# Token tiles for the channel stage turned by VectorE 32x32 blocks instead of TensorE transposes, with a new order at the stage's entry

## The chip, the core and the metric

One core of a Trainium2 chip. Time is device microseconds of the core, the median of three runs. The profile is of one execution, and its span runs from the first to the last instruction.

## What is computed

Windowed attention over 2 batches, 8 heads, 768 tokens, head size 64; then a gated unit (`w_in` 512x1024, a 768x768 product over tokens, `w_out` 512x512); then a low-rank token mix and a channel network (512 to 2048 to 512) with a residual:

```python
attn = softmax(scale * q @ k.T + bias, kept in the window) @ v     # -> x: 2 x 768 x 512
h = relu(x @ w_in); u, v = h[..., :512], h[..., 512:]
x2 = (u * (w_spatial @ layer_norm(v) + b_spatial)) @ w_out
u = x2 + (x2.T @ U @ V).T                                          # low rank, 32
out = u + relu(u @ w_ch1) @ w_ch2
```

All in float32. The kernel splits each operand of a large product in a high and a low part (`hi`, `lo`, type fp32r) and adds three products: hi by hi, lo by hi, hi by lo.

## The kernel before

Tokens lie in 12 tiles of 128 (6 of each batch), 512 columns each, in the SBUF tensor `tokens`. The engines run programs of their own, in an order written out by hand, and meet by semaphores. `wait(e, name, n)` adds a credit that the waiting side's buffers give.

Attention and the gated unit of batch 0 come first (`window`), then the in-products and layer norm of batch 1, then `finish`, which begins with `products(1)`: for each of its six tiles t TensorE runs `mix_tokens` (18 matmuls), six transposes of the next row of `w_spatial`, `low_rank(t-2)`, `project(t-1)` (12 matmuls), and the four transposes of the gated tile (`gate_transpose`, L1266). VectorE in the same period does `gate` (L957), two `wsp_lo`, `x2_lo(t-1)`, `gT_lo`; ScalarE the copies with the high parts. The gate of tile t must be done before `gate_transpose(t)`; `gT_lo(t)` before `project(t)`, one period later; `x2_lo(t)` before `low_rank(t)`, two periods later.

The channel stage works on groups of TB = 4 tiles, so there are NB = 3 groups. Each group needs its four tiles turned (`uT`, columns on partitions), split in `uT_hi` and `uT_lo`. Then it goes in NF = 16 steps: `hidden(n)` makes 128 of the 2048 hidden columns (12 matmuls of 512), ScalarE and VectorE split the result in `hT_hi` (L719) and `hT_lo` (L1094), and `down(n)` adds it into four y banks (12 matmuls). TensorE runs `hidden(n+1)` ahead of `down(n)`, and there are two buffers of h. After a group's last step VectorE adds y and tokens into `ys` (`y_out`, L1099), and SyncE stores it.

Before the change the tiles are turned in `u_transpose` (L1414): four TensorE transposes of a tile into one of two PSUM banks (2 and 3), then `uT_hi` on ScalarE (L712) and `uT_lo` on VectorE (L1089), both from PSUM. The first group's are set between the last products of batch 1: tiles 0 and 1 after `gate_transpose(5)`, tiles 2 and 3 after `project(5)`, and `hidden(0)` waits for all four. The second group's are set between `down(14)` and `down(15)`, the third's one group later. The third transpose of a group waits until the first bank has been split by both engines. The tokens of batch 1 are complete only after `add_low_rank(1, t)` (L983), which runs in the first steps of the first group, from `expand` (L1291).

Meanwhile GpSimd splits the channel weights (`split_chunk`, L402: a cast L408 and a subtraction L410 of 128x1024 for each chunk): eight chunks from 235 us on, the other eight after the last `gate`.

All of TensorE's products are at L1156, all its transposes at L1148, the two low-rank products at L1287, the expansion at L1297.

## Time and profile before

| | us |
|---|---|
| median of 3 runs | 570.76 |
| the three runs | 568.64, 570.76, 573.37 |
| the profiled execution | 568.82 |
| its span | 566.9 |
| TensorE busy in it | 532.1 (94%) |
| VectorE busy in it | 233.3 (41%) |
| ScalarE busy in it | 172.4 (30%) |
| GpSimd busy in it | 111.7 (20%) |

The granted TensorE clock is at full speed (2.4 GHz) in every one of the page's 40 slices. The channel stage runs from about 292 us to the end. A matmul of 128x512 shows about 390 ns in the trace, but back to back one starts every 0.227 us: matmuls are pipelined, so the starts tell the pace and the busy time does not. The same holds of VectorE on a smaller scale: a group of two rows can be shorter than twice the mean.

### The profile page before, as it was taken

To read this page: it belongs to the slowest core of one execution; us is meant where nothing else is said; L and a number is where in the kernel's file an instruction comes from. 1 tells how busy PE (TensorE), PEld (TensorE's weight loads), DVE (VectorE), ACT (ScalarE), POOL (GpSimd) and SP (SyncE) were. 2 spreads that over 40 slices of the span, in tenths; PEclk is the share of its full clock that TensorE was granted. 3 is DMA by queue.
4 is the path that set the end of the run, shared out by engine and by line. 5 is a ranking of instruction groups with operands and counts; after the bars stand their busy time and mean duration, and the time that the engine had idled before them with its cause. 6 is when DMAs were issued, how large, how long until landed. Compare 5 with 4: busy or idle time off the path is not lost.

```text
span 566.9 us, 7455 instructions
## 1 busy us (share of the span) xinstructions
PE 532.1 (94%) x2724; PEld 415.3 (73%) x2724; DVE 233.3 (41%) x656; ACT 172.4 (30%) x426; POOL 111.7 (20%) x134
## 2 busy tenths in 40 slices
PE   1789999889999999999979999999999999999996
PEld 0356666567777788778868888878888887888885
DVE  5668888867775436533343110123010114110112
ACT  2655665655555432223141011121011012011110
POOL 3786000000000001599299200000000000000000
PEclk9999999999999999999999999999999999999999
DMA  8995443545623000055133000001000002000002
GB/s 168 221 223 129 99 101 102 120 96 129 127 77 90 29 29 0 6 179 182 43 111 112 1 0 1 0 1 74 1 0 1 0 1 75 1 0 1 0 1 79
DMA packets 43977, 37.02 MB, mean 65 GB/s; under 512 B 25600, under 2 KB 37888, under 8 KB 43936
## 3 DMA queue, kind: packets, MB, share of 16 engines
q1 hardware_dynamic: 37920, 20.13, 16.3%
q0 software_dynamic: 3216, 11.63, 6.8%
q10 hardware_dynamic: 2800, 4.72, 2.9%
q8 instruction: 24, 0.39, 0.3%
q14 instruction: 17, 0.14, 0.1%
HBM read 33.33 MB, written 3.15 MB: 64 GB/s over the span
## 4 chain that ended last, share of the span: by engine, by line
PE 84%; DVE 5%; SPq 4%; issue 3%; DMA 2%; ACT 1%; POOL 0%; DVEq 0%; ACTq 0%; POOLq 0%
PE ps L1156 68%; PE ps L1148 6%; PE ps L1171 4%; PE ps L1196 4%; SPq L337 2%; DMA qk_even<-in_k 1%; PE ps L1287 1%; DMA wsp<-in_moe_w_spatial 1%; SPq L371 1%; DVE pr L869 1%; SPq L373 1%; DVE sc L853 1%; DVE gv_lo L937 1%; DVE q_turned L805 1%; POOL small L447 0%
## 5 line engine op out<-in xcount | busy, mean ns | idle before, releaser
L1096 DVE SCALAR_TENSOR_TENSOR hT_lo<-ps,hT_hi 128x512 fp32r<-128x512 f32 x48 | 33.2, 692 | 211.6 <-ACT hT_hi L722 211.6
L722 ACT ACTIVATE hT_hi<-ps 128x512 fp32r<-128x512 f32 x48 | 28.7, 598 | 224.9 <-PE ps L1156 224.9
L549 ACT ACTIVATE pr<-sc,small 128x256 f32<-128x256 f32 (+1 forms) x96 | 46.2, 482 | 52.9 <-DVE small L853 52.4
L1171 PE MATMUL ps<-k_turned,q_turned 64*128 64x256 f32 (+1 forms) x192 | 36.4, 460 | 16.4 <-DVE k_turned L805 10.0
L853 DVE CUSTOM_DVE_ANT_0 sc<-ps,bias 128x256 f32<-128x256 f32 (+1 forms) x96 | 34.9, 399 | 20.9 <-PE ps L1171 17.8
L1156 PE MATMUL ps<-win_hi,xT_hi 128*128 128x512 f32 x96 | 40.2, 419 | 0.0
L1156 PE MATMUL ps<-uT_hi,w1a_hi 128*128 128x512 f32 x96 | 37.5, 390 | 2.3 <-issue 2.3
L1156 PE MATMUL ps<-win_hi,xT_lo 128*128 128x512 f32 x96 | 37.7, 393 | 0.0
L1156 PE MATMUL ps<-w2b_hi,hT_hi 128*128 128x512 f32 x96 | 37.6, 392 | 0.0
L1156 PE MATMUL ps<-win_lo,xT_hi 128*128 128x512 f32 x96 | 37.5, 391 | 0.0
L1156 PE MATMUL ps<-w2b_hi,hT_lo 128*128 128x512 f32 x96 | 37.4, 390 | 0.0
L1156 PE MATMUL ps<-w2b_lo,hT_hi 128*128 128x512 f32 x96 | 37.4, 390 | 0.0
L1156 PE MATMUL ps<-uT_lo,w1a_hi 128*128 128x512 f32 x96 | 37.4, 390 | 0.0
L1156 PE MATMUL ps<-uT_hi,w1a_lo 128*128 128x512 f32 x96 | 37.4, 390 | 0.0
L1156 PE MATMUL ps<-w2a_lo,hT_hi 128*128 128x512 f32 x96 | 37.4, 390 | 0.0
L1156 PE MATMUL ps<-uT_hi,w1b_hi 128*128 128x512 f32 x96 | 37.4, 390 | 0.0
L1156 PE MATMUL ps<-uT_lo,w1b_hi 128*128 128x512 f32 x96 | 37.4, 390 | 0.0
L1156 PE MATMUL ps<-w2a_hi,hT_lo 128*128 128x512 f32 x96 | 37.4, 389 | 0.0
L1156 PE MATMUL ps<-uT_hi,w1b_lo 128*128 128x512 f32 x96 | 37.4, 389 | 0.0
L1156 PE MATMUL ps<-w2a_hi,hT_hi 128*128 128x512 f32 x96 | 37.4, 389 | 0.0
L1171 PEld LDWEIGHTS ps<-k_turned,q_turned 64*128 64x128 f32 x192 | 16.6, 211 | 26.0 <-DVE k_turned L805 10.0
L1148 PE MATMUL ps<-ident,pr 128*128 128x128 f32 x176 | 31.3, 301 | 3.8 <-issue 2.5
(144 smaller groups left out, 1052.8 us busy)
## 6 DMA issues: line engine op xcount, KB each, us to landing
w_raw<-in_moe_w_ch POOLq DMA_DIRECT2D x16, 512.0 KB, 4.1
wsp<-in_moe_w_spatial ACTq DMA_DIRECT2D x12, 384.0 KB, 3.3
vn<-in_v SPq DMA_DIRECT2D x12, 256.0 KB, 3.8
out<-ys SPq DMA_DIRECT2D x12, 256.0 KB, 2.3
qk_late<-in_q SPq DMA_DIRECT2D x24, 112.0 KB, 3.6
qk_late<-in_k SPq DMA_DIRECT2D x24, 112.0 KB, 3.8
vp<-in_v SPq DMA_DIRECT2D x10, 224.0 KB, 4.6
w_raw<-in_moe_w_in POOLq DMA_DIRECT2D x4, 512.0 KB, 7.5
```

What stands on the lines that cost most here:

```text
L337: e.dma_start(qk_in(tile)[rows, a, :, :, :].rearrange("p a n d -> p a (n d)"), src[head, tile // NT, tile % NT, :, :, x * TURN:(x + SPAN) ...
L371: sp.dma_start(vp[0:P - G, buf, :, :], v_d[b, i - 1, G:P, :, :]).then_inc(s[f"v_loaded{buf}"], 16)
L373: sp.dma_start(vp[P - G:P, buf, :, :], v_d[b, 0, 0:G, :, :]).then_inc(s[f"v_loaded{buf}"], 16)
L549: act.activation(pr[:, k % 3, e, 0:w], sc[:, k % 2, e, 0:w], ACT.Exp, bias=nmax[:, k % 2, e:e + 1], scale=-1.0, accum_out=sums[:, k % 3, e ...
L722: act.activation(hT[0][:, n % 2, :], h1_ps(n), ACT.Relu).then_inc(s["hT_hi"], 1)
L805: ins = dve.transpose(out.rearrange("p a (r c) -> p a c r", c=TURNS), qk_in(tile)[:, a, :, 0:SPAN:2, :])
L853: dve.tensor_tensor_reduce(out=sc[:, k % 2, e, 0:w], in0=scores_ps(e)[:, 0:w], in1=bias[:, 2 * p + e, WINDOW - w:WINDOW], scale=-SCALE, sc ...
L1096: dve.scalar_tensor_tensor(hT[1][:, n % 2, :], h1_ps(n), 0.0, hT[0][:, n % 2, :], ALU.max, ALU.subtract).then_inc(s["hT_lo"], 1)
L1148: return pe.transpose(dst, src, ident[:, :])
L1156: ins = pe.matmul(o, lhsT[a], r[c], start=first_of_bank and (a, c) == (0, 0), stop=last and (a, c) == (1, 0))
L1171: pe.matmul(scores_ps(e)[:, 0:w], q_turned[rows, tile % 2, p, :], keys[:, window_at(i):window_at(i) + w]).then_inc(s["scores"], 1)
L1196: ins = pe.matmul(x_ps(tile)[e * D:(e + 1) * D, p * P:(p + 1) * P], v[:, buf, 2 * p + e, :], probs[:, e, x * P:(x + 1) * P], start=x == 0, ...
```

## The change

The 48 TensorE transposes of `tokens` and the function `u_transpose` are gone. In their place VectorE runs `turn_tokens(n, x)`: for one block of 32 token partitions (x) it makes four block transposes, each from 32 partitions and 4 x 32 columns into another block of 32 partitions, so that four calls, 16 instructions, turn a tile of 128x512 wholly, from SBUF to SBUF. The turned float32 tile lies in `turned(n)`: for the first group in the place of `uT_lo`, for the other two in `ys[j]`. `uT_hi` and `uT_lo` now read it there instead of in PSUM.

When: the first group's four tiles in `products(1)`, periods t = 0 to 3, half of a tile ahead of `x2_lo(t-1)` and half behind `gT_lo(t)`; the second and third group's during the steps f = 5 to 12 of the group before, two calls (8 instructions) behind each `hT_lo`. ScalarE's `uT_hi` of the first group goes into periods 1 to 4, VectorE's `uT_lo` behind `gT_lo` of periods 2 to 5.

The order of TensorE at the entry becomes `low_rank(4)`, `hidden(0)`, `project(5)`, `hidden(1)`, `low_rank(5)`, `down(0)`, then the usual steps; the first `down` waits with its fourth column block for `mix_lo`, whose bank it takes over (y_ps 3 is now bank 1). `expand` and `add_low_rank` of batch 1 come one step later. `y_out` also waits for `uT_lo` of the next group, since both use `ys`; a turn of the third group waits for the store of the first group's output from the same buffer.

```diff
--- before.py
+++ after.py
...
+FIRST_TURN = 5
...
         uT = hi_lo("uT", [P, CM, TB * P])
+        uT_end = place[0]
+        place[0] = uT_at + CM * TB * P * 4
+        uT_first = sb("uT_first", [P, CM, TB * P])
+        assert place[0] == uT_end
...
-        def uT_ps(j):
-            return ps[:, 2 + j % 2, :]
+        def turned(n):
+
+            j = n % TB
+            return ys[j][:, :].rearrange("p (c n) -> p c n", c=CM) if n >= TB else uT_first[:, :, j * P:(j + 1) * P]
...
         def y_ps(j):
-            return ps[:, (0, 1, 5, 6)[j], :]
+            return ps[:, (0, 5, 6, 1)[j], :]
...
+            def uT_hi(tb, j):
+                if j == 0:
+                    wait(act, "h1_ps", tb * NF)
+                act.wait_ge(s["u_turned"], tb * TB + j + 1)
+                act.activation(uT[0][:, :, j * P:(j + 1) * P], turned(tb * TB + j), ACT.Copy).then_inc(s["uT_hi"], 1)
...
                     gT_hi(b, t)
+                    if b and 0 < t <= TB:
+                        uT_hi(0, t - 1)
...
-            def uT_hi(tb, j):
-                if j == 0:
-                    wait(act, "h1_ps", tb * NF)
-                wait(act, "u_transposed", tb * TB + j + 1)
-                act.activation(uT[0][:, :, j * P:(j + 1) * P], uT_ps(j).rearrange("p (c n) -> p c n", c=CM),
-                               ACT.Copy).then_inc(s["uT_hi"], 1)
...
             def finish():
                 products(1)
-                for j in range(2):
-                    uT_hi(0, j)
+                hT_hi(0)
                 x2_hi(1, NT - 1, True)
-                for j in range(2, TB):
-                    uT_hi(0, j)
-                hT_hi(0)
+                hT_hi(1)
                 mix_hi(1, True)
-                for n in range(1, NB * NF):
+                for n in range(2, NB * NF):
                     hT_hi(n)
...
+            def turn_tokens(n, x):
+
+                tb, j = n // TB, n % TB
+                wait(dve, "u_ready", n + 1)
+                if tb > 1:
+                    dve.wait_ge(s[f"stored{j}"], 16 * (tb - 1))
+                rows = tokens[x * TURN:(x + 1) * TURN, n, :].rearrange("p (c y r) -> p c y r", y=TURNS, r=TURN)
+                for y in range(TURNS):
+                    ins = dve.transpose(turned(n)[y * TURN:(y + 1) * TURN, :, x * TURN:(x + 1) * TURN], rows[:, :, y, :])
+                if x == TURNS - 1:
+                    ins.then_inc(s["u_turned"], 1)
+
+            def uT_lo(tb, j):
+                n = tb * TB + j
+                dve.wait_ge(s["uT_hi"], n + 1)
+                dve.tensor_tensor(uT[1][:, :, j * P:(j + 1) * P], turned(n), uT[0][:, :, j * P:(j + 1) * P],
+                                  ALU.subtract).then_inc(s["uT_lo"], 1)
+
             def products(b):
                 for t in range(NT):
                     gate(b, t, True)
                     for h in range(2):
                         if t + 1 < NT:
                             wsp_lo(b, t + 1, h, True)
+                    for x in range(2):
+                        if b and t < TB:
+                            turn_tokens(t, x)
                     if t:
                         x2_lo(b, t - 1, True)
                     gT_lo(b, t)
+                    for x in range(2, TURNS):
+                        if b and t < TB:
+                            turn_tokens(t, x)
+                    if b and t >= 2:
+                        uT_lo(0, t - 2)
...
-            def uT_lo(tb, j):
-                dve.wait_ge(s["uT_hi"], tb * TB + j + 1)
-                dve.tensor_tensor(uT[1][:, :, j * P:(j + 1) * P], uT_ps(j).rearrange("p (c n) -> p c n", c=CM),
-                                  uT[0][:, :, j * P:(j + 1) * P], ALU.subtract).then_inc(s["uT_lo"], 1)
...
                 if m >= TB:
                     dve.wait_ge(s[f"stored{j}"], 16 * (m // TB))
+                if m + TB < B * NT:
+                    dve.wait_ge(s["uT_lo"], m + TB + 1)
                 dve.tensor_tensor(ys[j][:, :], y_ps(j), tokens[:, m, :], ALU.add).then_inc(s["y_ready"], 1)
 
             def finish():
                 products(1)
-                for j in range(2):
-                    uT_lo(0, j)
+                hT_lo(0)
                 x2_lo(1, NT - 1, True)
-                for j in range(2, TB):
-                    uT_lo(0, j)
-                hT_lo(0)
                 mix_lo(1, True)
                 for n in range(1, NB * NF):
                     hT_lo(n)
-                    if n <= NT // 2:
-                        add_low_rank(1, 2 * n - 2)
-                        add_low_rank(1, 2 * n - 1)
-                    tb = (n + 1) // NF
-                    if n % NF == NF - 1:
+                    if 2 <= n <= NT // 2 + 1:
+                        add_low_rank(1, 2 * n - 4)
+                        add_low_rank(1, 2 * n - 3)
+                    tb, f = n // NF + 1, n % NF
+                    if tb < NB and FIRST_TURN <= f < FIRST_TURN + 2 * TB:
+                        for x in range(2):
+                            g = 2 * (f - FIRST_TURN) + x
+                            turn_tokens(tb * TB + g // TURNS, g % TURNS)
+                    if f == NF - 1:
...
                     if f == 0 and tb:
                         wait(pe, "y_ready", (tb - 1) * TB + j + 1)
+                    if n == 0 and j == TB - 1:
+                        wait(pe, "mix_split", B)
...
-            def u_transpose(tb, j):
-                n = tb * TB + j
-                wait(pe, "u_ready", n + 1)
-                wait(pe, "uT_lo", n - 1)
-                for c in range(CM):
-                    ins = transpose(uT_ps(j)[:, c * P:(c + 1) * P], tokens[:, n, c * P:(c + 1) * P])
-                ins.then_inc(s["u_transposed"], 1)
-
             def finish():
                 wait(pe, "u_ready", NT)
                 products(1)
                 wait(pe, "wspT_lo", 2 * B * NT)
-                for j in range(2):
-                    u_transpose(0, j)
                 low_rank(1, NT - 2, True)
+                hidden(0)
                 project(1, NT - 1, True)
-                for j in range(2, TB):
-                    u_transpose(0, j)
-                wait(pe, "gate", B * NT)
-                hidden(0)
+                hidden(1)
                 low_rank(1, NT - 1, True)
-                for n in range(NB * NF):
-                    tb = (n + 1) // NF
+                down(0)
+                for n in range(1, NB * NF):
                     if n + 1 < NB * NF:
                         if n % NF == NF - 1:
-                            for j in range(TB):
-                                u_transpose(tb, j)
                             down(n)
                             hidden(n + 1)
                             continue
                         hidden(n + 1)
-                    if n < NT // 2:
-                        expand(1, 2 * n)
-                        expand(1, 2 * n + 1)
+                    if n <= NT // 2:
+                        expand(1, 2 * n - 2)
+                        expand(1, 2 * n - 1)
                     down(n)
```

## Rows read from the trace of the kernel before

**Rows 1.** The page: busy time by engine, and the chain's shares of the span.

```profile
PE 532.1 (94%) x2724; PEld 415.3 (73%) x2724; DVE 233.3 (41%) x656; ACT 172.4 (30%) x426; POOL 111.7 (20%) x134
...
PE 84%; DVE 5%; SPq 4%; issue 3%; DMA 2%; ACT 1%; POOL 0%; DVEq 0%; ACTq 0%; POOLq 0%
```

**Rows 2.** Chain of waits at the second and third group: start us, us, what.

```profile
378.52 0.45 PE ps L1148 x4
...
381.74 87.11 PE ps L1156 x384
468.85 0.45 PE ps L1148 x4
...
472.35 89.81 PE ps L1156 x396
```

**Rows 3.** Chain of waits at the entry to the channel stage, same columns.

```profile
285.33 0.73 PE ps L1287 x2
...
289.83 2.27 issue
292.10 3.00 PE ps L1156 x12
295.10 0.45 PE ps L1287 x2
...
298.73 5.44 PE ps L1156 x24
```

**Rows 4.** Timeline of VectorE, 43 to 46 us: start us, us, engine, line, operation.

```profile
43.87 1.11 DVE L805 STREAM_TRANSPOSE q_turned<-qk_odd 128x512 f32<-128x512 f32 x1
44.82 1.10 DVE L805 STREAM_TRANSPOSE k_turned<-qk_odd 128x512 f32<-128x512 f32 x1
```

**Rows 5.** Groups of VectorE by form: xcount, busy us, mean ns, idle before.

```profile
L933 DVE TENSOR_SCALAR small<-small 128x1 f32<-128x1 f32 x12 | 1.8, 154 | 0.4
L937 DVE TENSOR_TENSOR gv_lo<-vnf,gv_hi 128x512 fp32r<-128x512 f32 x12 | 9.6, 800 | 1.7 <-ACT gv_hi L601 1.7
L980 DVE TENSOR_TENSOR mix<-ps,mix 32x512 fp32r<-32x512 f32 x2 | 1.4, 684 | 0.8 <-ACT mix L629 0.7
```

**Rows 6.** Timeline of VectorE, 237 to 286 us: the product stage of batch 1.

```profile
237.35 2.08 DVE L937 TENSOR_TENSOR gv_lo<-vnf,gv_hi 128x512 fp32r<-128x512 f32 x1 [0.70 <-ACT gv_hi L601]
...
246.46 0.75 DVE L964 SCALAR_TENSOR_TENSOR gated<-ps,small,gu 128x512 f32<-128x512 f32 x1 [3.13 <-PE ps L1156]
...
255.06 0.75 DVE L964 SCALAR_TENSOR_TENSOR gated<-ps,small,gu 128x512 f32<-128x512 f32 x1 [2.16 <-PE ps L1156]
255.91 1.02 DVE L956 TENSOR_TENSOR wspT_lo<-ps,wspT_hi 128x384 fp32r<-128x384 f32 x2
260.02 0.69 DVE L974 TENSOR_TENSOR x_lo<-ps,x_hi 128x512 fp32r<-128x512 f32 x1 [3.09 <-ACT x_hi L625]
...
285.19 0.68 DVE L969 TENSOR_TENSOR gT_lo<-ps,gT_hi 128x512 fp32r<-128x512 f32 x1
```

**Rows 7.** Timeline of GpSimd in the same stretch, same columns.

```profile
236.45 2.43 POOL L410 TENSOR_TENSOR w1a_lo<-w_raw,w1a_hi 128x1024 fp32r<-128x1024 f32 x1
...
266.81 1.05 POOL L408 CAST w2a_hi<-w_raw 128x1024 fp32r<-128x1024 f32 x1
267.94 2.40 POOL L410 TENSOR_TENSOR w2a_lo<-w_raw,w2a_hi 128x1024 fp32r<-128x1024 f32 x1
...
285.48 1.05 POOL L408 CAST w1b_hi<-w_raw 128x1024 fp32r<-128x1024 f32 x1
```

**Rows 8.** Chain of waits, 255 to 264 us: one tile of the product stage.

```profile
255.02 0.66 PE ps L1148 x6
...
256.14 2.73 PE ps L1156 x12
...
263.43 0.66 PE ps L1148 x6
```

**Rows 9.** Timeline of VectorE in the channel stage, 376 to 378 us.

```profile
376.46 0.69 DVE L1096 SCALAR_TENSOR_TENSOR hT_lo<-ps,hT_hi 128x512 fp32r<-128x512 f32 x1 [4.75 <-ACT hT_hi L722]
```

More of the change, by code:

```diff
@@ L63 @@
               pT_ready=2, av=1, xT_hi=1, xT_lo=2, d_xT_lo=3, v_relu=2, u_relu=2, wsp_transposed=1, wspT_lo=2, gate=2,
-              gT_lo=1, x2_split=2, low_rank=2, mix_split=1, h_ps=1, u_ready=2, u_transposed=1, uT_lo=2, h1_ps=1,
+              gT_lo=1, x2_split=2, low_rank=2, mix_split=1, h_ps=1, u_ready=2, h1_ps=1,
               hT_lo=2, h2=2, y_ready=4, d_bias=0)
@@ L201, in program @@
         place[0] = turned_at
+        uT_at = place[0]
         uT = hi_lo("uT", [P, CM, TB * P])
+        uT_end = place[0]
+        place[0] = uT_at + CM * TB * P * 4
+        uT_first = sb("uT_first", [P, CM, TB * P])
+        assert place[0] == uT_end
         hT = hi_lo("hT", [P, 2, TB * P])
@@ L292, in program @@
             x2_sum x2_hi x2_split low_rank mix_hi mix_split h_ps u_ready
-            u_transposed uT_hi uT_lo h1_ps hT_hi hT_lo h2 y_done y_ready""".split()}
+            u_turned uT_hi uT_lo h1_ps hT_hi hT_lo h2 y_done y_ready""".split()}
         def wait(e, name, n):
@@ L749, in _ @@
             give(dve, "qk_turned", "bias_ready", "biased", "normal", "xT_lo", "d_xT_lo", "wspT_lo", "gate", "gT_lo",
-                 "x2_split", "mix_split", "u_ready", "uT_lo", "hT_lo", "y_ready")
+                 "x2_split", "mix_split", "u_ready", "hT_lo", "y_ready")
             steps = [0]
@@ L1141, in _ @@
             give(pe, "low_rank", "scores", "probsT", "av", "wsp_transposed", "h_ps",
-                 "u_transposed", "h1_ps", "h2")
+                 "h1_ps", "h2")
             pe.wait_ge(s["dense_ready"], 1)
```

## The prediction

> **What bounds the kernel now.** I read the busy times of the page first, then the chain of waits over the second half of the span, then the timeline of each engine at the three places where tiles are turned. The busy times show TensorE at 532 of 567 us, VectorE at 233, and the chain lies on TensorE for 84% of the span [rows 1]. So an edit is worth what it takes off TensorE's own line or out of its idle time, and VectorE's added work costs nothing as long as it stays in VectorE's gaps. In the channel stage the chain is nothing but matmuls one behind another for 87 us between groups [rows 2]; it is broken only where tiles are turned. Those three places are the whole possible gain.
>
> **What is removed at the second and third group.** The chain leaves the matmuls at 378.52 and is back on them at 381.74, 3.22 us; at the next group 468.85 to 472.35, 3.50 us [rows 2]. Both stretches are the 16 transposes and a wait for the first PSUM bank to be split. After the change TensorE goes from `down(14)` to `down(15)` to `hidden(16)` with nothing between, if `uT` is ready. Is it? After `hidden(15)` the h split ends with `hT_lo` at 376.46 + 0.69 = 377.15 [rows 9]. Four `uT_lo` behind it, at 0.68 each and each fed by a ScalarE copy that is no slower, end by about 380; `hidden(16)` would start 12 matmuls (2.73, as in a `project` [rows 8]) behind 378.52, at 381.25. A margin of 1.2 us, so I take the whole 3.22 + 3.50 = 6.7 us as saved. The `y_out` that follow are needed only two products later.
>
> The turning itself puts 8 block transposes behind each `hT_lo` in steps 5 to 12. A step is 24 matmuls, 5.44 us [rows 3]; `hT_lo` takes 0.69 of it. The cover holds up to a price of (5.44 - 0.69) / 8 = 0.59 us for each block transpose; above it `hT_lo` falls back from step to step and `down` waits.
>
> **What one block transpose costs.** The trace has none of 32 partitions by 128 columns. The nearest are those of 128x512: 1.11 us long, and the next starts 0.95 behind [rows 4]. Fewer partitions give no rebate: a subtraction on 32 partitions took 0.684, as much as on 128 [rows 5, 6]. By columns: the lower bound is a quarter of the start distance, 0.24 us. If an instruction of one column takes 0.154 [rows 5] and the rest of 1.11 goes by columns, the length is 0.154 + 0.24 = 0.39. As a top I take 0.44, that length and a hand-over of 0.05 between two. The choice between 0.24 and 0.39 is whether the next one overlaps the tail of the one before. The transposes of the trace that overlap write the same partitions; the new ones change their output block with each instruction. I take 0.39.
>
> The Trainium skill, VectorE: DVE Perf Modes, section "Two Vector instructions with no wait between them", says that an instruction whose output starts in another group of 32 partitions than the one before begins only when all earlier ones have finished. No row of before shows such a pair; by that rule the overlap is gone in all 192 instructions, and the price is at or above the full length. The same page's section "The three transpose paths" gives 311 ns for 128 columns of 16-bit data and advises TensorE for a full 128x128 transpose; by its figure the entry below would come out as in the cheap case, about -9 in all.
>
> **The entry, without VectorE's load.** In before the chain ends `down(0)` 2.72 into the piece that starts at 298.73, at 301.45, of which 0.45 are two expansions that now come later: 301.0 [rows 3]. After: `low_rank(4)` still waits for `x2_lo(4)` until 285.33, now idle, and ends at 285.8. `hidden(0)` waits for `uT_lo(3)`, which stands behind `gT_lo(5)` (to 285.87 [rows 6]). That subtraction now has two SBUF inputs, and here is a cost that it did not have from PSUM: `gv_lo` of the same shape, started during a GpSimd subtraction, took 2.08, where the other eleven have a mean of (9.6 - 2.08) / 11 = 0.68 [rows 5], and ended 0.55 behind that instruction's end [rows 6, 7]. GpSimd's cast runs from 285.48 to 286.53 [rows 7], so `uT_lo(3)` ends at 287.1. Then `hidden(0)` 2.75, `project(5)` 2.73, `hidden(1)` 2.73, `low_rank(5)` 0.47, `down(0)` 2.72: 298.5. `mix_lo` is done by about 297.3 and its user is the last quarter of `down(0)`, at 297.8. Saving 2.5 us. Of the old waits, 2.27 us ahead of 292.10 and a short one ahead of 285.33, the latter stays and grows by the eight transposes that filled its front, and 1.3 us are left ahead of `hidden(0)`.
>
> **VectorE's load in `products(1)`.** A period is 8.41 us (255.02 to 263.43 [rows 8]). VectorE's work in it is `gate` 0.75, `wsp_lo` 1.02, `x2_lo` 0.69, `gT_lo` 0.68, and from the third period on `uT_lo` 0.68: 3.8 us. Added in periods 0 to 3: 16 block transposes, 3.8 us at 0.24, 6.2 at 0.39, 7.0 at 0.44. So up to 0.28 the period holds them (3.8 + 4.5 = 8.3); at 0.39 it is overfull by 1.6 in a period with `uT_lo`. What comes late is the next `gate`, queued behind the turns, and TensorE waits for it at `gate_transpose`, 0.66 + 0.45 + 2.73 = 3.84 behind the end of `mix_tokens` [rows 3, 8], less 0.75 for the gate: 3.1 us of slack. Step by step at 0.39 (one half turn 3.1 us):
> - t=1: gate at 249.1 instead of 246.46, done 249.9, TensorE needs it at 250.4. `wsp_lo` to 250.8, half turn, `x2_lo` to 254.5, `gT_lo` to 255.1, half turn.
> - t=2: gate at 258.2 instead of 255.06, done 258.9: TensorE loses up to 0.3. Then half turn, `x2_lo` to 263.6, `gT_lo` to 264.2, half turn to 267.3, and `uT_lo(0)` meets the cast of 266.81 to 267.86 [rows 7] and ends at 268.4.
> - t=3: gate 268.4 to 269.1: TensorE loses 1.7. The same again, without a GpSimd instruction in the way: `uT_lo(1)` to 278.0.
> - t=4: gate done 278.7: loses 1.2. No turns any more; by t=5 nothing waits.
>
> Sum of losses 3.2, and GpSimd's second half, started by the last gate, shifts along with it. The entry is then -2.5 + 3.2 = about +0.8 us (with rounding). Total: -6.7 + 0.8 = **-5.9 us**. Against the profiled span 566.9 that is 561.0; laid on the median of before, 570.76, it is 564.9. The profiled execution (568.82) lies 1.9 below that median, and I assume the same pace for after.
>
> Hidden and at no cost: ScalarE's `uT_hi` from SBUF (ScalarE is idle for 70% of the span [rows 1]), the waits of `y_out` for `uT_lo` (long done, same engine), those of the turns for the stores (three quarters of a group earlier), the swap of y banks.
>
> **The rivals.**
> - Cheap block transposes (price at most 0.36): losses in the products vanish or stay under 1 us; the entry gives -2.5 to -1.6 and the total is -9.3 to -8.4, so 561.5 to 562.4. For it: the start distance of rows 4. Against: outputs in other partitions each time.
> - Dear ones (0.41 to 0.48). The same walk at 0.44 loses 0.5, 1.4, 2.6 and 2.0 us, above all because `uT_lo(0)` now falls in the GpSimd subtraction of 267.94 to 270.34 [rows 7] and drags the gate behind it. Entry +4.0, total -2.7: 568.1. The skill's rule of the held instruction leads here if the hand-over is added to the length.
> - Slower than before: VectorE becomes the bound. From 0.50 the walk's loss (+7.3) eats the 6.7; from 0.59 the steps of the channel stage fall behind too. At 0.60 the entry loses some 13.7, total +7: 578. It needs a price above half of a four times longer one; little speaks for it.
> - The gain at the group boundaries doesn't come whole: `uT_lo` of the second group is later than `hidden(16)`, by more than the 1.2 us of margin, say because ScalarE's four copies come at 0.9 instead of 0.5 each. It would give back up to 2 us of each boundary: total -2, 568.9.
>
> **How the numbers follow.** Forecast case (price 0.37 to 0.40) 0.33, cheap 0.30, dear 0.27, boundaries late 0.05, slower 0.05. The three first are one mechanism at three prices, and the time forecast lies between them. A difference under 1%, 5.7 us, can't be told from no change here. Faster by over 1%: all of the cheap case and 0.25 of the forecast case, 0.55. Within 1%: the rest, 0.40. Slower 0.05. The range goes from the cheap case with 1 us for the spread of a median, 560.5, to the dear one with 2.7, 570.8.
>
> **What would show it.** Right: no transposes of `tokens` on TensorE, an unbroken chain of matmuls over both boundaries (each 3.2 to 3.5 shorter), block transposes starting 0.39 apart, the gates of t=3 and t=4 late by 1 to 2 us against TensorE, `hidden(0)` behind a `uT_lo` that ends after a GpSimd instruction. Wrong: block transposes under 0.3 or over 0.42 apart; `uT_lo` that is not held by GpSimd; a granted clock under full speed after one of the waits in the product stage, which before's gap of 2.27 us did not cause.

## The result and the profile after

| | before | after |
|---|---|---|
| median | 571.84 us (4 runs, 568.64 to 573.37) | 564.01 us (4 runs, 561.43 to 565.52) |
| span of the profiled execution | 566.9 | 559.6 |
| VectorE busy | 233.3 | 292.0 |
| TensorE busy | 532.1 | 525.5 |

The ratio is 0.9873 with a 95% interval of 0.9844 to 0.9902: 1.3% faster. The forecast was 564.9 us, a saving of 5.9; measured is a saving of 7.8 between these medians and of 7.3 between the two profiled spans.

The page of the kernel after, its parts 1 and 2 and one group of part 5 (busy us, mean ns of one | idle before):

```profile
PE 525.5 (94%) x2676; PEld 409.6 (73%) x2676; DVE 292.0 (52%) x848; ACT 172.2 (31%) x426; POOL 112.1 (20%) x134
...
PEclk9999999999999999999989999999999999999999
...
L1003 DVE STREAM_TRANSPOSE ys<-tokens 32x128 f32<-32x128 f32 x128 | 38.7, 302 | 1.8
```

VectorE has taken on 58.7 us of work, 192 block transposes at 0.302 us and little else, and the span fell all the same: the work went into its gaps. One digit of the clock is new, the 8 in the 21st slice, which is the entry to the channel stage. In [rows 1] the chain lay on TensorE for 84% of the span; now it is 80%, because it runs over VectorE in the products of batch 1. The chain of waits of after over 255 to 480 us (start us, us, what):

```profile
263.50 2.40 DVE uT_lo L1010
265.90 0.67 DVE gated L970
...
284.47 0.69 DVE x_lo L980
285.16 0.60 DVE gT_lo L975
285.76 1.21 DVE uT_lo L1010
...
287.01 10.09 PE ps L1185 x36
297.10 0.45 PE ps L1316 x2
297.55 5.44 PE ps L1185 x24
...
315.23 164.79 PE ps L1185 x727
```

Three things are to be read in it. The last row runs to the end of the window, at 480: where [rows 2] had 3.22 and 3.50 us of turning and waiting, matmuls now follow each other without a break. The first row is `uT_lo(0)`, which took 2.40 us instead of 0.68 and made a gate late. And `hidden(0)`, `project(5)` and `hidden(1)`, the 36 matmuls from 287.01, take 10.09 us where 36 at the usual distance of 0.227 take 8.2.

What TensorE waited for in after from 225 us on (us in total, times, longest):

```profile
PE ps L1316 <- DVE x_lo L980: 1.6, 1, 1.6
PE ps L1185 <- DVE gv_lo L943: 1.1, 1, 1.1
PE ps L1185 <- DVE uT_lo L1010: 1.0, 1, 1.0
PE ps L1177 <- DVE gated L970: 0.8, 2, 0.6
```

VectorE's timeline in the products of after, a few of its rows:

```profile
241.73 2.50 DVE L1003 STREAM_TRANSPOSE uT_first<-tokens 32x128 f32<-32x128 f32 x8
...
263.50 2.40 DVE L1010 TENSOR_TENSOR uT_lo<-uT_first,uT_hi 128x512 fp32r<-128x512 f32 x1
265.83 0.74 DVE L970 SCALAR_TENSOR_TENSOR gated<-ps,small,gu 128x512 f32<-128x512 f32 x1
...
285.68 1.28 DVE L1010 TENSOR_TENSOR uT_lo<-uT_first,uT_hi 128x512 fp32r<-128x512 f32 x1
```

and GpSimd's in the same stretch:

```profile
262.96 2.40 POOL L418 TENSOR_TENSOR w2a_lo<-w_raw,w2a_hi 128x1024 fp32r<-128x1024 f32 x1
...
285.35 1.05 POOL L416 CAST w1b_hi<-w_raw 128x1024 fp32r<-128x1024 f32 x1
```

Eight block transposes take 2.50 us: one is 0.302 long and they start 0.315 apart. Both slow `uT_lo` end 0.5 us behind the end of the GpSimd instruction (265.90 and 286.96 against 265.36 and 286.40), as `gv_lo` did before [rows 6, 7].

**Where the 7.3 us of the two spans lie.** In both kernels TensorE waits for `gv_lo` ahead of the last three matmuls of batch 1's first `mix_tokens`; the entry is counted from there, for all kernels below too, to the start of `down(0)`. Before took 239.49 to 298.73 [rows 3], less 0.45 for two expansions that come later now, so 58.8. After took 238.92 to 297.55, 58.6: the entry gained 0.2. From `down(0)` to the last matmul, with the two expansions counted alike, it gained 6.8, the 6.7 of the boundaries and 0.1; the end behind the last matmul took 0.25 longer. The other 0.6 us lie ahead of 239, where the two programs have the same work and single executions begin this stretch anywhere from 238.9 to 241.8. Part of that spread goes with the clock: the six of this document's fourteen profiles with a granted clock of 0.83 to 0.85 from 110 to 120 us begin it at 239.98 to 241.81, the other eight at 238.88 to 240.05.

Before's 58.8 holds a chance delay. This row of TensorE's timeline of before is a wait for a row of `w_spatial` to land:

```profile
246.84 0.88 PE L1148 MATMUL ps<-ident,wsp 128*128 128x128 f32 x6 [0.41 <-DMA wsp<-in_moe_w_spatial]
```

The other profiles of before (`before_b` and `before_c`, below) don't have it, nor has after; with the slower start behind it, it puts TensorE 0.65 us back by the next `project`. `before_c`, at full clock and without it, has an entry of 58.1. So the gain is the boundaries, and the entry is a wash: 0.2 us better than this execution, 0.5 worse than one without the late load. The questions for the chip were why, and whether it must be.

### The profile page after: what moved, and what is told of

Same layout as the page of the kernel before. It is cut to its first block, busy times and chain, and to the rows that moved or that the text cites. A ratio compares the mean times of both kernels' runs of the same rounds, so it can differ in the third digit from the quotient of the medians.

```text
span 559.6 us, 7557 instructions
## 1 busy us (share of the span) xinstructions
PE 525.5 (94%) x2676; PEld 409.6 (73%) x2676; DVE 292.0 (52%) x848; ACT 172.2 (31%) x426; POOL 112.1 (20%) x134
## 4 chain that ended last, share of the span: by engine, by line
PE 80%; DVE 9%; DMA 3%; POOL 3%; issue 3%; ACT 1%; SPq 0%; DVEq 0%; POOLq 0%; ACTq 0%
PE ps L1185 66%; PE ps L1177 5%; PE ps L1225 4%; PE ps L1200 4%; DMA w_raw<-in_moe_w_in 3%; DVE uT_first L1003 2%; POOL win_lo L433 2%; PE ps L1316 1%; DMA qk_even<-in_q 1%; POOL win_hi L431 1%; DVE pr L875 1%; DVE uT_lo L1010 1%; DVE wspT_lo L962 1%; DVE gv_lo L943 1%; DVE sc L859 1%
## 5 line engine op out<-in xcount | busy, mean ns | idle before, releaser
L1003 DVE STREAM_TRANSPOSE ys<-tokens 32x128 f32<-32x128 f32 x128 | 38.7, 302 | 1.8
```

The lines of the kernel that those rows point to most:

```text
L1003: ins = dve.transpose(turned(n)[y * TURN:(y + 1) * TURN, :, x * TURN:(x + 1) * TURN], rows[:, :, y, :])
```

## Experiments

The theories at this point. **Load:** VectorE's 64 block transposes in the products make gates late, by their price and by `uT_lo` meeting GpSimd. **Clock:** the two waits at the entry (1.6 and 1.0 us, with only the two matmuls of `low_rank(4)` between them) bring TensorE to its lower clock, and the next matmuls pay. The profile has a sign of it. TensorE's timeline of after behind the second wait:

```profile
288.58 0.63 PE L1185 MATMUL ps<-uT_lo,w1a_hi 128*128 128x512 f32 x1
289.01 0.63 PE L1185 MATMUL ps<-uT_hi,w1a_lo 128*128 128x512 f32 x1
289.43 0.63 PE L1185 MATMUL ps<-uT_hi,w1a_hi 128*128 128x512 f32 x1
```

and its windows (from:to, us, busy time and count of PE, PEld, DVE, ACT and POOL, then the granted clock, the DMA share and GB/s):

```profile
287.00:288.00 1.00, 0.99 (x3) 0.85 (x4) 0.00 (x0) 0.00 (x0) 1.00 (x1) 0.70 0.70 270
288.00:289.00 1.00, 1.00 (x3) 0.72 (x3) 0.00 (x0) 0.00 (x0) 1.00 (x1) 0.50 0.03 12
289.00:290.00 1.00, 1.00 (x4) 0.80 (x3) 0.00 (x0) 0.00 (x0) 0.70 (x2) 0.50 0.00 0
290.00:291.00 1.00, 1.00 (x5) 0.76 (x3) 0.00 (x0) 0.00 (x0) 1.00 (x2) 0.59 0.15 33
```

The matmuls start 0.427 apart instead of 0.227, and the granted clock is half, 1.2 GHz, until shortly before 291.

### The changed kernel once more, and the boundaries alone

`after_again` is the changed kernel, unedited, measured beside the next three.

> The changed kernel itself once more, beside the experiments. Both theories: 0.983 to 0.991 of before, a span about 7 us shorter. If the half clock that its profile showed from 287.2 to 290.7 us comes from the two waits of TensorE just ahead of it (1.56 and 1.00 us with two matmuls between), it is there again in this profile, at the first hidden product. If it was an accident of one execution, it is not.

Measured: 562.44 us, ratio 0.9865 [0.9835, 0.9896], span 559.7. The 36 matmuls took 10.06 us, and the entry was 58.6 again. In this profile TensorE also waited 0.42 us for `w_spatial`, as in before, but then not for the gate of t=3: 0.6 us back, it found the gate just done. The two delays overlap instead of adding up.

`e3_later_groups` turns the first group with TensorE, in the old order; only the second and third go to VectorE:

```diff
+            def u_transpose(n):
+                if n >= 2:
+                    pe.wait_ge(s["uT_lo"], n - 1)
+                for c in range(CM):
+                    ins = transpose(uT_ps(n)[:, c * P:(c + 1) * P], tokens[:, n, c * P:(c + 1) * P])
+                ins.then_inc(s["u_transposed"], 1)
...
-                    for x in range(2):
-                        if b and t < TB:
-                            turn_tokens(t, x)
```

> Only the second and third group are turned by VectorE; the first group is turned by TensorE in the old order at the entry. Theory (all of the gain is at the two group boundaries, the entry gained nothing): 6.7 us less than before, as fast as the changed kernel or up to 0.5 us slower, 0.988 of before. Rival, as I had predicted the cheap case (the entry gives 2.5 us too): 2.5 us slower than the changed kernel.

Measured: 563.62 us, 0.9873 [0.9851, 0.9896]: most of the gain of the whole change, which measured beside it is 1.2 us faster (`after_again`), between the theory's 0 to 0.5 and the rival's 2.5. The chain of waits of this kernel at the entry:

```profile
290.60 0.87 PE ps L1182 x8
291.48 2.27 issue
293.75 4.57 PE ps L1190 x12
```

The boundaries carry nearly all of the gain. But here is something that the profile of before had not shown: the same wait of 2.27 us stood in [rows 3], and behind it `hidden(0)` took 3.00 us; here the same 12 matmuls took 4.57. The half clock can fall on the old entry too. With it on both sides, this entry takes 60.2 us, from 241.81 to `down(0)` at 301.99, and the changed one 59.1 (58.6 and the two expansions): the new entry by itself is worth about 1 us.

### The clock and the order

`e1_order` takes away what makes TensorE wait. `uT_lo(3)` goes ahead of `x2_lo(4)` on VectorE, and `hidden(0)` ahead of `low_rank(4)` on TensorE, so that `hidden(0)` covers the splitting of `x2(4)`:

```diff
+                    if b and t == NT - 1:
+                        uT_lo(0, TB - 1)
                     if t:
                         x2_lo(b, t - 1, True)
...
-                    if b and t >= 2:
+                    if b and 2 <= t < NT - 1:
                         uT_lo(0, t - 2)
...
+                hidden(0)
                 low_rank(1, NT - 2, True)
-                hidden(0)
```

> uT_lo of the fourth tile goes ahead of x2_lo(4) on VectorE, where VectorE idles for 3.5 us, and hidden(0) ahead of low_rank(4) on TensorE. Both waits of TensorE at the entry then have hidden(0) in their place. Theory (the waits cost themselves and the half clock behind them): 1.56 + 1.00 us of waits and 9 matmuls x (0.427 - 0.227) = 1.8 us of clock go, 4.4 us less than the changed kernel, about 0.980 of before, clock full through the entry. Rival (the half clock has another cause): only 2.6 us less, and the half clock stays somewhere in hidden(0) or project(5).

Measured: 559.10 us, 0.9806 [0.9784, 0.9828], span 557.0. Its chain at the entry:

```profile
285.63 2.77 PE ps L1187 x12
288.39 0.45 PE ps L1318 x2
288.85 5.44 PE ps L1187 x24
...
294.74 5.44 PE ps L1187 x24
```

Neither wait is left, and no slow matmul: 54.0 us for the entry (from 240.71), 4.6 less than after. The median fell by 3.3 against `after_again`, and the profiled span by 2.7, because in this execution the entry began 1.8 us later than there; that stretch was not touched.

`e2_fill` keeps both waits and gives TensorE something to do in them: six matmuls on weights that lie there anyway, into a free bank, in front of `low_rank(4)`, and four in front of `hidden(0)`.

```diff
+                for _ in range(6):
+                    pe.matmul(ps[:, 2, :], wout[0][:, 0, 0:P], wout[0][:, 0, :])
                 low_rank(1, NT - 2, True)
+                for _ in range(4):
+                    pe.matmul(ps[:, 2, :], wout[0][:, 0, 0:P], wout[0][:, 0, :])
                 hidden(0)
```

> Ten matmuls of 128x512 that nobody reads go into TensorE's two waits at the entry, 6 ahead of low_rank(4) (1.36 us) and 4 ahead of hidden(0) (0.91 us). They fill the waits and should not lengthen them. Theory (the half clock comes from TensorE standing idle): the clock stays full, 1.8 us less than the changed kernel. Rival (cause elsewhere): same time as the changed kernel, half clock as before.

Measured: 560.97 us, 0.9841 [0.9819, 0.9862], span 558.6. The chain has the waits as they were, and behind them:

```profile
286.27 1.23 DVE uT_lo L1010
...
287.55 8.45 PE ps L1185 x36
```

8.45 us instead of 10.09, and 57.0 us for the entry, 1.6 less. Of the two things that `e1_order` removed, the clock is worth 1.6 us and the waits the rest, 3.0 (their idle time is 1.56 and 1.00, and by the starts each delays the work behind it by 0.25 more). That the filling is what kept the clock up is not shown by this one profile: the count below has profiles at full clock with the waits unfilled.

Is it certain that the clock falls there? `before_b` and `before_c` are the kernel before, unedited, each in a profile of its own.

> The kernel before, profiled again. It has a wait of 2.27 us ahead of hidden(0); its first profile showed a full clock behind it, the experiment with the old entry order (e3_later_groups) a half clock for the same wait. Theory (whether the chip answers such a wait with the half clock differs from one execution to the next): of three profiles of before, one or two show hidden(0) at about 4.6 us instead of 2.7. Rival (before never has it): 2.7 to 3.0 us in all.

> The same kernel and question as before_b, a third profile: hidden(0) at 4.6 us (half clock) in one or two of the three by the theory, at 2.7 to 3.0 us in all by the rival.

Measured: 572.31 and 570.38 us. The chain of `before_b`:

```profile
291.39 2.27 issue
293.66 4.57 PE ps L1156 x12
```

and that of `before_c`:

```profile
291.36 2.27 issue
293.63 3.01 PE ps L1156 x12
```

The same wait, to a hundredth, with half clock in one and not in the other. The entry of `before_c` (241.70 to 300.26) is the 58.1 us used above, at full clock; after less its 1.6 for the clock is 57.0, so at full clock too the new entry is worth about 1 us. Counting all profiles: of the old entry two of four have it (`before_b` and `e3_later_groups`; not before, not `before_c`). Of the entry with waits of 1.6 and 1.0 us four of six have it (after, `after_again`, and `e4`, `e5` below; not `e6`, `e9` below). So it comes in some executions and not in others at either entry, at 1.6 us when it comes; what decides is not shown. Whether the new entry has it more often, so few profiles don't tell. Of the four profiles in which these waits are filled or gone (`e1_order`, `e2_fill`, and `e10`, `e8` below) none has it. That speaks for the waits as its cause, against six of ten with them, though each of the four alone would prove little.

`e10_before_fill` fills the old wait with nine matmuls on the kernel before:

```diff
+                pe.wait_ge(s["chunk_split"], ready["ch1", 0])
+                for _ in range(9):
+                    pe.matmul(ps[:, 5, :], w1[0][0][:, 0, 0:P], w1[0][0][:, 0, 0:4 * P])
                 wait(pe, "gate", B * NT)
                 hidden(0)
```

> The kernel before with nine matmuls (2.04 us) that nobody reads in its wait of 2.27 us ahead of hidden(0). Theory (the half clock also strikes before, in a part of the executions): full clock behind the wait, and a median 0.5 to 1.8 us below before, 0.997 to 0.999, at the edge of what can be measured. Rival (before never pays it): the same time as before or 0.1 us more.

Measured: 570.39 us against 571.09, 0.9988 [0.9970, 1.0006] over 12 runs against 17. Its chain:

```profile
290.02 2.10 PE ps L1434 x9
...
292.29 3.01 PE ps L1156 x12
```

`hidden(0)` is at full speed in this profile, but it was so in half of those without the filling (two of four), and the time is inconclusive: a gain of some half of 1.6 us is no larger than the interval. For the old entry the use of filling was not shown.

### The price of a block transpose, and the load

`e4_same_block` writes each block to the partitions that it comes from, so output partitions no longer change from one transpose to the next within a call. Its tokens are therefore turned block by block only, and the blocks of a tile are not exchanged.

```diff
-                    ins = dve.transpose(turned(n)[y * TURN:(y + 1) * TURN, :, x * TURN:(x + 1) * TURN], rows[:, :, y, :])
+                    ins = dve.transpose(turned(n)[x * TURN:(x + 1) * TURN, :, y * TURN:(y + 1) * TURN], rows[:, :, y, :])
```

> The block transposes write into the block of partitions that they read (the turned tile is wrong: blocks are turned but not exchanged), so that the four of one call read and write the same partitions. Theory (a change of the output partitions holds the next instruction until the one before has finished): inside a call of four the starts are 0.25 us apart or less, against 0.315 in the changed kernel, at the same length of 0.302; between calls, where input and output block change, still 0.315. Rival (0.315 is what an instruction of 128 columns takes anyway): 0.315 throughout.

One execution: 561.75 us, span 559.8. VectorE's timeline and the group of these transposes (min/median/max ns):

```profile
242.77 1.76 DVE L1003 STREAM_TRANSPOSE uT_first<-tokens 32x128 f32<-32x128 f32 x8
...
L1003 DVE STREAM_TRANSPOSE uT_first<-tokens x64: 256/260/307, 242.8 to 271.4; 32x128 f32<-32x128 f32 x64
```

Eight in 1.76 us instead of 2.50. Inside a call the starts are 0.19 to 0.23 apart, so each overlaps the one before; where the next call begins, on other partitions, it is 0.28. The length, which the theory had left at 0.302, is 0.26 in the middle, so 0.28 is again just behind the end of the one before. In after every start comes 0.013 us behind the end of the one before. The Trainium skill, VectorE: DVE Perf Modes, section "Two Vector instructions with no wait between them", says this of instructions whose output starts in another group of 32 partitions; the trace agrees, 0.315 against 0.19 to 0.23. The entry took 57.8 us here with the half clock in it (the 36 matmuls 10.08), 0.9 less than after.

`e6_one_turn` turns a whole tile with one instruction of 128x512, which turns each block in its place (its blocks are not exchanged either):

```diff
...
-                for y in range(TURNS):
-                    ins = dve.transpose(turned(n)[y * TURN:(y + 1) * TURN, :, x * TURN:(x + 1) * TURN], rows[:, :, y, :])
...
+                if x < TURNS - 1:
+                    return
+                ins = dve.transpose(turned(n).rearrange("p c (y r) -> p c y r", r=TURN),
+                                    tokens[:, n, :].rearrange("p (c y r) -> p c y r", y=TURNS, r=TURN))
```

> One transpose instruction of 128x512 for each tile instead of 16 (1.1 instead of 5.0 us; blocks are turned in place but not exchanged between partitions, so the output is not the reference's). This takes nearly all of the new load off VectorE. Theory (at 0.315 the load costs TensorE only the late gates): the product stage and the entry are 0.5 to 1 us shorter than the changed kernel's, no more, and the half clock behind the two entry waits stays. Rival (the load costs much more, 3 us as I had reckoned): 3 us shorter.

One execution: 559.65 us, span 557.8. The group, and the chain behind the same two waits:

```profile
L1003 DVE STREAM_TRANSPOSE uT_first<-tokens x4: 701/702/703, 243.6 to 269.3; 128x512 f32<-128x512 f32 x4
...
286.70 8.46 PE ps L1185 x36
```

The entry took 55.9 us, 2.8 less than after: 1.6 is the clock, which stayed up this time (10.09 against 8.46), and 1.15 is the load, the `uT_lo(0)` that it pushed into GpSimd's subtraction with it. That is all that VectorE's transposes in the products cost the changed kernel. TensorE's starts show where: counted from the start of the entry, the `mix_tokens` behind the gate of t=3 begins at 28.26 in after and 27.29 here, 0.97 later, and the one behind the gate of t=4 at 36.86 and 35.70, 1.16 later. That second gate ended at 275.16 in after, 0.06 ahead of TensorE's first transpose, too close for it to run on at the usual pace; the four transposes took 0.56 us to the next matmul instead of 0.35.

And a surprise: 0.70 us for 128x512, where the transposes of [rows 4] have 1.11. Those write with a stride. `e9_stride` is `e6_one_turn` with its output elements 16 bytes apart, into the same tile (so those too are in other places than the reference's):

```diff
-                ins = dve.transpose(turned(n).rearrange("p c (y r) -> p c y r", r=TURN),
+                ins = dve.transpose(turned(n).rearrange("p c (r y) -> p c y r", r=TURN),
```

> As e6_one_turn, but the 32 columns of each block are written 4 elements (16 bytes) apart, as the transposes of q and k write them. Theory (what made the transposes of q and k take 1.11 us for 128x512, where e6's take 0.70, is the stride of the output): 1.11 here. Rival (it is the input, which in q and k is read in pieces of 32 columns with gaps): 0.70. The output is not the reference's.

One execution: 560.71 us. The group:

```profile
L1003 DVE STREAM_TRANSPOSE uT_first<-tokens x4: 1089/1092/1100, 244.4 to 270.2; 128x512 f32<-128x512 f32 x4
```

The stride alone turns 0.70 into 1.09. Its entry, at full clock, is 55.9 us as in `e6_one_turn`.

`e5_double` issues the first group's block transposes twice, the second set into spare space:

```diff
+                for y in range(TURNS if n < TB else 0):
+                    dve.transpose(spare[y * TURN:(y + 1) * TURN, n, :, x * TURN:(x + 1) * TURN], rows[:, :, y, :])
```

> In the first group each block transpose is issued twice (once into a spare place), so a tile costs 32 x 0.315 = 10.1 us instead of 5.0. Theory (VectorE's load in the products is at its limit, and what is late is the gate): my walk with 0.63 in place of 0.315 has gates late against TensorE by 3.0, 3.0, 3.6 and 3.6 us in the tiles 1 to 4, and a time 15 to 18 us above the changed kernel, about 579. Rival (the turns have slack, the gate is not what binds): under 5 us more.

One execution: 581.96 us, span 580.0, 20.4 more than after. What TensorE waited for:

```profile
PE ps L1184 <- DVE gated L975: 12.8, 5, 3.4
```

The theory had 15 to 18 us, for gates late by 3.0 to 3.6; they were late by 2.9 to 3.4, and the time is above it. The added 64 instructions come to 20.2 us at 0.315, and the span grew by just that. Its chain of waits says why. From 241 to 293.9 us it lies on VectorE alone, one instruction behind another with 0.01 to 0.03 us between most of them; around the gate of t=1 it reads:

```profile
252.47 0.31 DVE uT_first L1010
...
252.81 0.75 DVE gated L975
253.56 0.93 DVE wspT_lo L967 x2
```

At this load VectorE is the bound of the products, and each added transpose counts in full. The mechanism is the one of the prediction's walk (the gate queued behind the turns, TensorE behind the gate), now five times up to 3.4 us instead of twice up to 0.6. The waits are only 12.0 us more, since TensorE also ran slower between them: the granted clock was 0.83 of full speed in four of the six stretches of 10 us from 240 on, where after has 1.00 in all up to 280. That slow clock lies beside VectorE's chain and so adds nothing there of its own.

### A better version

`e8_best` is `e1_order` with `uT_lo(0)` and `uT_lo(1)` one period later and the last two in front of `x2_lo(4)`, so that none delays a gate of a period that still has turns:

```diff
                     if b and t == NT - 1:
+                        uT_lo(0, TB - 2)
                         uT_lo(0, TB - 1)
...
-                    if b and 2 <= t < NT - 1:
-                        uT_lo(0, t - 2)
+                    if b and 3 <= t < NT - 1:
+                        uT_lo(0, t - 3)
```

> As e1_order, and each uT_lo of the first group one period later (periods 3, 4, and the last two in period 5 ahead of x2_lo(4)), where GpSimd stands still, so that none is held by GpSimd's subtraction. Theory (uT_lo(0) held for 2.40 us delays the gate of tile 3 and TensorE behind it by 0.2 to 0.7 us, as in the changed kernel's profile): 0.3 to 0.7 us less than e1_order, 0.979 to 0.980 of before. Rival (that wait is covered elsewhere, or the two uT_lo ahead of x2_lo(4) meet GpSimd's cast): the same time as e1_order.

Measured: 556.98 us (5 runs, 556.25 to 557.64) against 570.26, ratio 0.9767 [0.9746, 0.9787], span 555.3. Its chain:

```profile
284.47 2.77 PE ps L1188 x12
287.23 0.45 PE ps L1319 x2
...
293.58 5.44 PE ps L1188 x24
```

and VectorE's timeline:

```profile
281.56 2.12 DVE L1010 TENSOR_TENSOR uT_lo<-uT_first,uT_hi 128x512 fp32r<-128x512 f32 x2
```

The entry is 53.5 us, 0.5 under `e1_order`. But 0.4 of that is the late load of `w_spatial`, which both profiles have: TensorE waits 0.82 us for it in `e1_order` and 0.48 here. That delay also hid what the edit is for. In `e1_order` `uT_lo(0)` was held as in after, to 267.71, but the gate behind it ended at 268.37 and TensorE, itself late, needed it only at 268.84. So the theory's 0.3 to 0.7 us is not shown by this pair of profiles, and the 2.1 us between the medians are not explained. Two `uT_lo` still meet a GpSimd instruction (2.12 us for the pair instead of 1.3), but now nothing waits for them. It is the fastest of all kernels here, 2.3% under before and 1.1 points under the changed kernel; it takes 5.3 us off before's entry of 58.8 (both with the late load), and the boundaries' 6.7.

## Why the prediction came out

The time, 564.01 against 564.9, is as forecast, but two terms at the entry are off, the load and the clock, and they nearly cancel. The savings agree less well: before's median rose from 570.76 to 571.84 with its fourth run, so the saving was 7.8 us between these medians, also 7.8 for `after_again` beside its own runs of before, and 7.3 between spans, against 5.9. To that extent the number was luck.

- **The boundaries, -6.7.** Right in place and size. The worry was `uT_lo` behind `hT_lo`. VectorE's timeline of after shows it in good time:

```profile
375.74 0.69 DVE L1123 SCALAR_TENSOR_TENSOR hT_lo<-ps,hT_hi 128x512 fp32r<-128x512 f32 x1 [4.75 <-ACT hT_hi L731]
376.35 2.49 DVE L1010 TENSOR_TENSOR uT_lo<-ys,uT_hi 128x512 fp32r<-128x512 f32 x4
```

  Four of them took 2.49 us, against 4 x 0.68 in the forecast, and began 0.61 behind the start of `hT_lo`, where [rows 9] had led me to 0.69. They ended at 378.84, 1.5 us ahead of `hidden(16)` at 380.35, where the forecast had a margin of 1.2. The cover in steps 5 to 12 held too: 8 x 0.315 and a `hT_lo` fill 3.2 of 5.44 us.
- **The price of a block transpose.** Forecast 0.39, measured 0.315. The order of events was right: each waits for the one before, as the changed output partitions make it. The step that failed is the quarter of 1.11 us for the columns: it was read from transposes that write with a stride [rows 4], and the new ones write side by side. A contiguous 128x512 takes 0.70 (`e6_one_turn`); with the fixed 0.154 of [rows 5], a quarter of the rest gives 0.154 + 0.137 = 0.29, against 0.302 measured, so the fixed part was about right. The hand-over, put at 0.05 for the dear case, is 0.013. The 311 ns that the Trainium skill gives for 16-bit data in VectorE: DVE Perf Modes, section "The three transpose paths", and that I had left outside the sum, was the nearest figure of all. The Trainium skill's rule of the held instruction agrees with the trace (0.315 against 0.19 to 0.23, `e4_same_block`). The rival that I had built on it did not come: I had added a hand-over to a length that was itself too long.
- **The load in the products, +3.2.** Mis-sized by this price: 1.15 us by `e6_one_turn`. (The walk's own times give 3.0, not 3.2: the gate of t=4 done at 278.7, needed at 275.7.) Redone at 0.315 the prediction's walk loses 0.13 us in all, so it is too low at the true price. TensorE waited 0.6 us for the gate of t=3 behind `uT_lo(0)`, which GpSimd held to 265.90, and with the slower start behind that wait lost 0.97; the gate of t=4 cost the other 0.2. That it would be held was foreseen (for a cast, and it was a subtraction), and `e5_double` shows the walk's mechanism at a load where it decides.
- **The entry without load, -2.5.** `e6_one_turn`, at full clock and nearly without load, has 55.9 us against 58.8: -2.9. But 0.65 of it is before's late load of `w_spatial`; against `before_c`, 58.1, it is -2.2, and the forecast lies between. `uT_lo(3)`, forecast to end at 287.1 behind GpSimd's cast, ended at 286.96.
- **The clock, not in the sum.** +1.6 us. The prediction named a clock under full speed as what would show it wrong, and set it aside since before's gap of 2.27 us had not caused it. This is the step that failed in kind: one execution had been taken for a rule. The next profiles of the same kernel have it in one of two, behind the same wait.

At the entry these make -2.9 + 1.15 + 1.6 = -0.2, as in the accounting, where the forecast had +0.8; without the late load it is -2.2 + 1.15 + 1.6 = +0.5. By its price alone this was the prediction's cheap case, with a total of -8.4 to -9.3; the half clock brought it back towards the forecast one. The other rivals did not come: no dear transposes, no VectorE as the bound, no late boundaries. The 1.4 us by which the spans fell more than forecast are the 1.0 at the entry, of which 0.65 is the late load, and 0.6 ahead of it, where nothing was changed, less 0.1 behind. The medians of before differ by more than a microsecond from one measurement to the next (570.2 to 571.84), so nothing finer can be read from them.

## What to carry to other kernels

Turning tiles on an engine with idle time pays where the turning stood alone on TensorE's line, here between groups; where it is queued in front of the work that TensorE waits for, count each period of that engine with the price, and place the turns and the splits that follow behind what is waited for (`e8_best` is some 6 us faster than the change by order alone). Price an instruction by a row with the same access pattern: a stride in the output made the transposes 56% longer here (1.09 against 0.70). And a wait of TensorE of 1 to 2.3 us can cost more than its length, by a clock that falls behind it in some executions (1.6 us here). So look at several profiles before a gap is called harmless, and let independent work run in its place. The same goes for any difference below a microsecond between two profiles: a late load moved before's entry by 0.65.

## What the runs showed of the hardware

- A wait of 2.27 us on TensorE, or two of 1.6 and 1.0 us with two matmuls between them, was followed by a granted clock of 0.5 in 6 of 10 profiles, and not in the others, with the same waits. The matmuls of 128x512 then start 0.427 us apart instead of 0.227; it costs 1.6 us. The Trainium skill, TensorE: Matmul & The Clock Gate, section "Wait — 56ns, not 53.3ns?", gives 426.7 ns for a clock of 1.2 GHz, with which the trace agrees, and 215.7 at 2.4 GHz, where this kernel has 227. The lower clock was absent in all four profiles whose waits were filled with matmuls or gone (`e2_fill`, `e10_before_fill`, `e1_order`, `e8_best`); the time of `e2_fill` was 1.5 us less than that of `after_again`.
- A transpose of 128x512 fp32 from SBUF to SBUF took VectorE 0.70 us into adjacent elements and 1.09 into elements 16 bytes apart. One of 32x128 took 0.302 us, and the next began 0.315 behind its start when its output lay in another block of 32 partitions, 0.19 to 0.23 in the same one (`e4_same_block`, length 0.26).
- A VectorE subtraction with both inputs in SBUF, 0.68 us alone, took 1.28 and 2.40 when a GpSimd instruction was running at its start, and ended 0.5 us behind it. It goes both ways: a GpSimd cast that began at 282.87 in `e1_order`, during such a subtraction (282.72 to 283.40), took 1.43 us instead of 1.05. One with an input in PSUM kept its 0.69 (259.62, `x2_lo`, during the subtraction of 258.41 to 260.81). The block transposes, with one input, kept their 0.315 under the same GpSimd instructions (257.11 to 259.61, during the subtraction of 258.41 to 260.81).
